# A tile's attention products regrouped on TensorE, with four buffers of turned probabilities and the sink columns packed earlier

## What is computed

```python
# B, H, S, D = 4, 8, 768, 64; n_sink, window = 4, 128
scores = q @ k^T / sqrt(D)
keep = (key < n_sink) | (0 <= query - key < window)
a = exp(scores - max) / (sum + 1e-9)            # over the kept keys
x = (a @ v) reshaped to 3072 tokens x 512
logits = x @ w_gate                             # 8 experts
y = gate * relu(x @ w1[e]) @ w2[e]              # e = argmax(logits)
h = y @ w_in;  out = (h - tanh(h)) @ w_out
```

## Time and profile before

| | |
|---|---|
| median of three runs | 1126.31 us (1126.26 to 1127.74) |
| the profiled execution | 1127.19 us |
| its span, first to last instruction | 1125.4 us |
| PE busy | 1090.5 us, 97% of the span |
| DVE, ACT, POOL busy | 54%, 43%, 44% of the span |
| first scores | at 4.58 us |
| last product of the score passes, then the tail | from 183.15 us |
| experts begin (their first slot's weights meet the tokens) | at 207.56 us |
| mean granted clock of TensorE | 0.990 of full |

### The profile page before, as it was taken

How to read it: one execution, slowest core, us unless ns; L and a number is a source line. 1 busy time by engine, 2 the same in 40 slices (tenths; PEclk the granted TensorE clock), 3 DMA queues, 4 the chain that set the end, 5 groups by cost and what they waited for, 6 DMA issues and landing times.

```text
span 1125.4 us, 17079 instructions
## 1 busy us (share of the span) xinstructions
PE 1090.5 (97%) x5993; PEld 870.8 (77%) x5993; DVE 611.1 (54%) x1326; ACT 478.8 (43%) x1016; POOL 491.3 (44%) x494
## 2 busy tenths in 40 slices
PE   8999998799999999999989999999999999999995
PEld 5766765588888888888867888888888888888884
DVE  5787777232223222322258666666666666666664
ACT  6788875324233424351354333333333333333331
POOL 3246625617016345483175335335335335435432
PEclk9999999899999999999999999999999999999998
DMA  7545832534215243464241100001010010000000
GB/s 255 196 129 172 269 108 95 169 121 148 86 57 188 94 159 122 139 217 159 66 132 57 31 17 38 19 20 38 10 29 38 1 38 38 1 1 38 1 1 38
DMA packets 37916, 99.44 MB, mean 88 GB/s; under 512 B 8272, under 2 KB 8400, under 8 KB 32720
## 3 DMA queue, kind: packets, MB, share of 16 engines
q1 hardware_dynamic: 29392, 52.30, 15.0%
q0 software_dynamic: 8448, 46.17, 11.9%
HBM read 75.84 MB, written 22.61 MB: 87 GB/s over the span
## 4 chain that ended last, share of the span: by engine, by line
PE 88%; DVE 5%; POOL 3%; issue 2%; ACT 1%; DMA 1%; POOLq 0%; DVEq 0%; SPq 0%; ACTq 0%
PE bank L676 22%; PE bank L668 21%; PE bank L604 14%; PE bank L618 14%; PE bank L462 4%; PE bank L428 3%; PE bank L444 2%; PE bank L610 2%; DVE prob L932 1%; PE bank L591 1%; POOL weights L1299 1%; PE bank L656 1%; POOL sq L1389 1%; PE bank L504 1%; PE bank L494 1%
## 5 line engine op out<-in xcount | busy, mean ns | idle before, releaser
L1299 POOL TENSOR_TENSOR weights<-raw,weights 128x1024 fp32r<-128x1024 f32 x72 | 171.3, 2399 | 201.7 <-ACT weights L724 201.1
L668 PE MATMUL bank<-mT_hi,weights 128*128 128x512 f32 x768 | 252.2, 390 | 1.7 <-DVE mT_lo L1126 1.7
L676 PE MATMUL bank<-weights,gT_hi 128*128 128x512 f32 x768 | 242.7, 397 | 5.6 <-DVE gT_lo L1183 5.4
L1388 POOL TENSOR_SCALAR ser<-ser 128x512 f32<-128x512 f32 x96 | 63.8, 665 | 286.7 <-DVE ser L1165 286.6
L676 PEld LDWEIGHTS bank<-weights,gT_hi 128*128 128x128 f32 x768 | 142.7, 190 | 39.6 <-DVE gT_lo L1183 11.0
L668 PEld LDWEIGHTS bank<-mT_hi,weights 128*128 128x128 f32 x768 | 144.4, 188 | 32.0 <-DVE mT_lo L1126 2.0
L676 PE MATMUL bank<-weights,gT_lo 128*128 128x512 f32 x384 | 150.9, 393 | 0.0
L604 PE MATMUL bank<-weights,mT_hi 128*128 128x512 f32 x464 | 148.0, 400 | 1.5 <-issue 1.5
L668 PE MATMUL bank<-mT_lo,weights 128*128 128x512 f32 x384 | 149.5, 389 | 0.0
L618 PE MATMUL bank<-weights,hT_hi 128*128 128x512 f32 x464 | 148.7, 401 | 0.0
L875 ACT ACTIVATE bank<-bank 128x512 f32<-128x512 f32 x96 | 55.9, 582 | 213.9 <-DVE ser L1175 213.9
(11 more groups left out here) (141 smaller groups left out, 1577.8 us busy)
## 6 DMA issues: line engine op xcount, KB each, us to landing
raw<-w_all POOLq DMA_DIRECT2D x32, 1024.0 KB, 5.5
raw<-w_all SPq DMA_DIRECT2D x8, 1024.0 KB, 7.0
sorted_y<-ys SPq DMA_DIRECT2D x30, 257.0 KB, 3.3
xs<-sorted_x SPq DMA_DIRECT2D x29, 257.0 KB, 2.8
kT<-kt SPq DMA_DIRECT2D x24, 264.0 KB, 2.8
qT<-qt SPq DMA_DIRECT2D x24, 256.0 KB, 3.2
v_in<-vt SPq DMA_DIRECT2D x24, 256.0 KB, 3.8
raw<-sorted_y SPq DMA_DIRECT2D x20, 257.0 KB, 2.7
```

The costliest lines, as they stand in the source:

```text
L668: done = e.matmul(bank[HB[n % 3]][:, :], wt[:, f // 2, c, cols], x[:, c, :], start=(c == 0 and m == 0), stop=(c == CH - 1 and m == 2))
L676: done = e.matmul(bank[YB[i]][:, :], x[:, n % 3, rows], wt[:, f, :], start=(f == 0 and m == 0), stop=(f == GCH - 1 and m == 2))
L1299: e.tensor_tensor(lo, src, hi.bitcast(F32), ALU.subtract).then_inc(s_w_lo, 1)
L1388: e.tensor_scalar(row, row, SERIES_2, 1.0, ALU.mult, ALU.add).then_inc(s_ser, 1)
```

## The change

On TensorE a pass now runs scores of two pairs, the last two turns of tile g, the sinks' turn, scores of the other two pairs, and then all four pairs' values of tile g in one piece. `logits` and `turn_x` of tile w follow, then `sink_values`, and the first two turns of tile i with `turn_logits` between them. Before, the values of pair 0 stood at the end of pass i and those of pairs 1, 2 and 3 at three places of pass i + 1. `probT` has four buffers, one for each pair, so `part` waits for the same pair's values of the tile before. The turned output takes its place in the order of banks ahead of the first turn of tile i. ScalarE and VectorE follow the new order, and `pack_sinks` and `guard_sums` run on GpSimd at the end of the pass that computed the probabilities, ahead of that pass's `split_lo`, not at the beginning of the next. The space for the buffers is taken from an unused gap (`ZEROS_AT`).

```diff
@@ order of the PSUM banks of turns
         if 0 <= g < ALL:
             turns += [("prob", g, 2), ("prob", g, 3)]
-        if i < ALL:
-            turns += [("prob", i, 0)]
         if 0 <= w < ALL:
             turns += [("x", w, 0)]
         if i < ALL:
-            turns += [("prob", i, 1)]
+            turns += [("prob", i, 0), ("prob", i, 1)]
...
-        probT = sb("probT", [P, 2, 2, 2, P], F32, arena)
+        probT = sb("probT", [P, PAIRS, 2, 2, P], F32, arena)
@@ TensorE, pass i
                 if i < ALL:
                     scores(i, 0)
                     scores(i, 1)
                 if in_values:
-                    values(g, 1)
                     turn_prob(g, 2)
                     turn_prob(g, 3)
...
                 if sinks:
                     turn_sinks(g)
-                if 0 <= w < ALL:
-                    logits(w)
-                if in_values:
-                    values(g, 2)
-                if w == ALL - 1:
-                    keep_warm(2)
-
                 if i < ALL:
                     scores(i, 2)
                     scores(i, 3)
                 if in_values:
-                    values(g, 3)
+                    for p in range(PAIRS):
+                        values(g, p)
+                if 0 <= w < ALL:
+                    logits(w)
+                    turn_x(w)
+                if w == ALL - 1:
+                    keep_warm(2)
+                if sinks:
+                    sink_values(g)
                 if i < ALL:
                     turn_prob(i, 0)
-                if sinks:
-                    sink_values(g)
                 if 0 <= w < ALL:
                     turn_logits(w)
-                    turn_x(w)
                 if i < ALL:
                     turn_prob(i, 1)
-                    values(i, 0)
@@ part, on ScalarE and on VectorE
-                if PAIRS * g + p >= 2:
-                    e.wait_ge(s_values, PAIRS * g + p - 1)
+                if g:
+                    e.wait_ge(s_values, PAIRS * (g - 1) + p + 1)
@@ ScalarE, pass i
                 if i < ALL:
-                    exp(i, 0)
-                    exp(i, 1)
-                    exp(i, 2)
-                    exp(i, 3)
+                    for h in range(3):
+                        exp(i, h)
                 if in_values and part_on_act(g, 3):
                     part(g, 3)
                 if in_values and g % TILES > 1:
                     sinks_evict(g)
+                if i < ALL:
+                    for h in range(3, H):
+                        exp(i, h)
...
                 if 0 <= w < ALL:
                     logits_evict(w)
...
                 if in_values:
                     o_evict(g)
-                if i < ALL:
-                    exp(i, 7)
-                    if part_on_act(i, 1):
-                        part(i, 1)
+                if i < ALL and part_on_act(i, 1):
+                    part(i, 1)
@@ VectorE, pass i
-                    if h in (2, 3) and in_values and not part_on_act(g, h):
-                        part(g, h)
+                    if h == 3 and in_values:
+                        for p in (2, 3):
+                            if not part_on_act(g, p):
+                                part(g, p)
                     next(routing, None)
+                if 0 <= w < ALL:
+                    normalise(w)
                 if i < ALL:
                     part(i, 0)
                 if 0 <= w < ALL:
                     add_logits(w)
-                    normalise(w)
@@ GpSimd, pass i
-                if i - 1 in sink_count:
-                    pack_sinks(i - 1)
-                if 0 <= i - 1 < ALL:
-                    guard_sums(i - 1)
...
+                if i in sink_count:
+                    pack_sinks(i)
+                if i < ALL:
+                    guard_sums(i)
                 for g in to_scatter:
                     scatter(g)
                 if 8 <= i < 16:
                     split_lo(0, i - 8)
```

More of the change, by code:

```diff
@@ L49, in build @@
     QW = 2048
-    ZEROS_AT = 1700
+    ZEROS_AT = 676
     HW = QW // 2
@@ L462, in values @@
                         done = e.matmul(bank[O_BANK][n * D:(n + 1) * D, p * P:(p + 1) * P],
-                                        v_in[:, tile % RING_V, h * D:(h + 1) * D], probT[:, p % 2, n, side, :],
+                                        v_in[:, tile % RING_V, h * D:(h + 1) * D], probT[:, p, n, side, :],
                                         start=(p == 0 and side == sides[0][0]), stop=(t < 2 and p == PAIRS - 1 and side == 1),
@@ L501, in logits @@
                 e.wait_ge(s_oT, w + 1)
+                if w + 1 in sink_count:
+                    e.wait_ge(s_sinkT, sink_count[w + 1])
                 each = P // PAIRS
@@ L737, in part @@
                 e.wait_ge(s_turned, PAIRS * g + p + 1)
[L738 to L740 removed]
+                if g:
+                    e.wait_ge(s_values, PAIRS * (g - 1) + p + 1)
+                e.activation(probT[:, p, :, :, :].rearrange("p n s c -> p (n s c)"), bk[:, :],
                              ACT.Copy).then_inc(s_part_act, 1)
@@ L744, in sinks_evict @@
                 e.wait_ge(s_sink_turned, sink_count[g])
-                e.wait_ge(s_logits, g)
                 if g - 2 in sink_count:
```

23 lines of the change are left out of this document (7 added, 16 removed).

## The result

| | before | changed |
|---|---|---|
| median, first timing (13 runs each) | 1126.88 us (1124.81 to 1127.74) | 1124.49 us (1123.80 to 1126.93) |
| median, second timing (17 and 11 runs) | 1127.11 us (1124.40 to 1127.77) | 1124.03 us (1122.39 to 1125.09) |
| ratio, 95% interval | | 0.9984 (0.9976 to 0.9991), then 0.9979 (0.9970 to 0.9987) |
| profiled execution, its span | 1127.19 us, 1125.4 us | 1124.74 us, 1123.0 us |
| last start of scores | 174.90 us | 171.69 us |

The changed kernel is faster, by 2.4 us in one timing and 3.1 in the other by the medians (1.8 and 2.4 by the ratios), where some 8 were forecast. The sign was right, the size wrong by a factor of about three. The gain up to the first expert product was 3.93 us, half of the forecast, and not all of that shows at the end.

What follows compares the result with a forecast made beforehand. TensorE, busy 171.7 of 178.6 us, was taken as the bound. Terms 1.9 + 0.3 + 1.4 + 0.4 + 0.15 + 2.3 + 1.9 - 0.4 = 7.95 us off 1127.19 gave 1119.2, median 1118, range 1112 to 1124.5.

Steps and rivals of the forecast that it cites:

- a change of form: On TensorE, each leaving of a 64- or 32-wide form costs 0.16 or 0.17 us; three values pieces save 0.48 per pass.
- four pairs' values: On TensorE in an inner pass, the grouped values piece takes 0.59 + 3 x 0.43 = 1.88 us.
- the two new transitions: On TensorE, scores to turns and sinks to scores, taken at no extra cost; bounds 0 and 0.17 us each.
- the second scores: On TensorE, the second score piece waits for mask rows to free its banks: 0 to 0.2 us, taken as 0.1.
- passes 0 and 1: In the first two passes, the 0.9 us wait for `oT` goes and form changes give 1.0: 1.9 us less.
- the packing: Passes 11 and 12 lose 1.9 us of waits for packed sinks, plus 0.4 for what stands behind: 2.3 us less.
- Nothing net in the routing passes: Passes where VectorE also routes: 0.4 us less, against 0.4 more from GpSimd's later split; 0.0 together.
- a net loss of 0.2 in two passes (9 and 15): GpSimd's later split holds a small VectorE step of the gates: 0.4 us more in all.
- The wait is 0.14: In an inner pass, TensorE's second turn waits for `normalise`: 1.38 us from the turned output's start against 1.24 of work.
- 6.48 us for a pass with t = 1: Three passes with t = 1 fall from 6.94 to 6.48 us, 0.46 each, 1.4 less.
- The stage's gain reaches the end in full: The experts follow a chain that starts when routing ends, so all 7.95 us of the score stage's gain reaches the end.
- the new waits eat the form gain: Rival: inner passes stay at about 7.5 us; 4.7 us less or down to 3, 1121.5 to 1123; chance 0.16.

Runs made afterwards that it cites:

- experiment 2: Changed kernel with the values of pairs 0 and 1 put ahead of the second scores on TensorE; 1123.11 us in one run.
- experiment 4: Two kernels: kernel before with packing and guarded sums moved to the pass's end, 1126.58 us; changed kernel with them put back, 1125.42 us.
- experiment 5: Changed kernel with GpSimd's weight pieces in passes 9 to 13 and 15 to 17, 1125.19 us; the same with the turned output ahead of logits, 1122.47 us.
- experiment 6: Changed kernel, turned output ahead of logits, routing steps behind last mask rows: weight pieces moved as in experiment 5 1121.35 us, unmoved 1121.40, only pass 13's moved 1120.38.
- Experiment 3: Changed kernel with the turned output ahead of the logits on TensorE; 1121.17 us in one run, then 1122.17 us in the median of 5.
- experiment 1: Changed kernel with GpSimd's pieces of weights right after a pass's first merge, not after the packed sinks; 1126.94 us.

## Why the prediction was wrong

Right were the bound, the sign, and most prices: 0.16 to 0.17 for a change of form (0.15 in experiment 2); 1.88 for four pairs' values (1.90); nothing for the two new transitions; 0.1 for the second scores; 1.9 for passes 0 and 1 (2.04); 2.3 for the packing (2.30, and 2.3 again in experiment 4, though with the new order in place only 1.6 of it hang on the packing, and the order itself gives the other 0.7). Of the 7.95 us forecast up to the first expert product 4.0 are missing. Four steps failed, all in the part on the change; the first three make 4.5 us, and the tail and the first passes gave 0.5 back.

- **Nothing net in the routing passes, and "a net loss of 0.2 in two passes (9 and 15)".** Measured 2.36 us, the largest error. The step that failed was that the delayed piece of weights would meet the gates' step alone. It met that one (0.43 and 0.47 for passes 9 and 15 instead of 0.2 each), and the piece of pass 13 met the sinks' low half too, a step that I had not looked for: 1.30 us in pass 14. Experiments 4, 5 and 6 show cause and size: without the late piece pass 14 takes 8.57 or 8.58 and passes 9 and 15 take 7.81 and 7.84, and moving one piece takes 1.29 off pass 14. The rest is that 8, 20 and 21 gain nothing and lose 0.1, 0.1 and 0.2, where 0.1 each was to be gained. Mask rows late behind routing steps delay their second scores, about as forecast, and experiment 6 takes 0.3 off; what was to be gained at the second turn did not come, since that still stands 1.51 us and more behind the turned output. Passes 9 and 15 were given no form gain, with no reason said; without the late piece they show none (7.81 and 7.84 against 7.81 and 7.77), so this was luck.
- **"The wait is 0.14".** It was 0.27: `normalise` starts 0.76 after the turned output and not 0.64. In eight inner passes and the three with t = 0 the forecast was off by 1.4 + 0.4 us, most of it by this. Experiment 3 takes the wait away and gets 7.37 us. The hand-over was read from a row of two turns, 0.04 us behind the modelled end, and the length of 0.60 from a turned output with other work behind it; here the row lasts 0.66 and `normalise` starts 0.10 behind its end.
- **6.48 us for a pass with t = 1.** It took 6.62 to 6.65, mostly by the same 0.13. The turned logits do wait 0.20 for ScalarE's copy in each of the three (0.6 in the waits above), but within the 1.51 us that the second turn waits for `normalise` anyway.
- **"The stage's gain reaches the end in full".** The chain carries it in the first profiled execution, to 567 us; in the second, 0.75 us of it went in the experts. And a gain of this size is of the order of what one execution loses or wins by the clock's fall at the last stage's entry, 1.2 to 1.6 us. The profiled pair of the result had it on one side only.

The rival "the new waits eat the form gain" came closest: it gave 1121.5 to 1123 with inner passes near 7.5, which is what they took. But its 3 to 4.7 us holds the measured 3.93 by luck: it left about 0.5 us for everything but the packing and the start (1.0 was measured for t = 1 alone), and it missed the routing passes too, by as much as my sum. The rule of the Trainium skill that I weighed ("SBUF — State Buffer", section "SBUF: two separate sides": an instruction of VectorE with two SBUF inputs, or in a mode that uses two ports, and one of GpSimd exclude each other, the later waits for the other to end) would have given 1120.5, nearer than my sum. The rows agree with it at every place that was found: 62.53 against 62.46, 65.78 against 65.77, 66.69 against 66.68, each the end of the held step and of the piece; the sinks' low half ends 0.55 us behind its piece (104.02, 103.47), a little less than its own 0.68. The gates' step has one SBUF input, so by this page it would have to be in such a mode, which no row shows. I had applied it to the one step of the trace that showed it already, and not to every VectorE step that the later piece would pass.

## What to carry to other kernels

When a change moves a long GpSimd instruction, list every VectorE step that would then begin during it and either has two inputs in SBUF or is a copy, cast or product by a scalar from SBUF to SBUF, and price each at the rest of the piece; a piece moved away from one often meets the next (experiments 1 and 6), so the whole pass has to be looked through, and the queue that waits for the piece's slot as well (experiment 5). When work is grouped to save changes of form, look first at what the grouped block leaves between a product and the reader of its bank: of the 0.48 us saved here 0.27 + 0.10 came back as waiting, and one exchange of two neighbours recovered 0.13. A gain of 2 to 3 us in 1125 is not much more than one fall of the clock (1.2 to 1.6); compare it at an event ahead of that place, and time it often.

## What the runs showed of the hardware

- A VectorE step beside GpSimd's 2.37 us piece was held to the piece's end when it read two SBUF tiles (0.20 to 1.92; the sinks' low half 0.68 to 1.88, ending 0.55 behind it) or was a TENSOR_SCALAR or a CAST from SBUF to SBUF (0.17 to 1.05 and 1.86, 0.16 to 2.35). RECIPROCAL and TENSOR_REDUCE from SBUF kept their 0.20 and 0.27 us, mask rows and products out of PSUM their 0.43 and 0.69. Where the sinks' low half had begun first (104.71, experiment 4), it took 0.71 us and the piece behind it 2.64.
- Changes of form on TensorE cost 0.14 to 0.17 us where one side is 64 or 32 wide, and less than 0.1 between 128 x 128 and 96 x 128 (four of the latter took 0.48 us from start to start, four of 128 x 128 0.41).
- The granted clock at 565 to 575 us was 0.83 in one execution of the changed kernel and 1.00 in another with the same wait of 1.89 us ahead of it; at that place it cost 1.6 us. Eight of the nine executions without this fall have one of 3.4 us later, between 576.6 and 586.6 us, and it shows no cost (541.7 to 541.8 us from the reload to the end, and the same in the ninth, which has neither fall). In another kernel it fell behind a wait of 0.84 us in one execution (1.3 us for the values alone) and not behind one of 0.83 in another.
